# A float32 pipeline of attention and two weighted layers: six places for the row tiles of w_out, and a new order of seeds and sums at the borders and in the later experts

## The chip, the core and the metric

The kernel runs on one core of a Trainium2 chip. The metric is the device time of one execution in microseconds. The engines are named as in the profile: PE is the matrix engine (PEld its weight loads), DVE the vector engine, ACT the scalar engine, SP the queue from which all transfers are issued.

## The reference

Attention within chunks of 64 positions gives a matrix x of 2304 tokens by 512. A gated layer follows, and then four experts, weighted by probabilities:

```python
x = attention(q, k, v)                       # softmax(q k^T / 8) v, in chunks of 64
x = (x @ w_a * (x @ w_b)) @ w_out            # 512 -> 1536 -> 512
p = probs / (probs.sum(-1) + 1e-9)
for e in range(4):
    out += p[:, e] * (relu(x @ w1[e]) @ w2[e])   # 512 -> 1024 -> 512
```

All of it is float32. The 2304 tokens are worked in three thirds of 768.

## The kernel before

**Precision.** Each float32 operand is split into a rounded part (HI, written by ACT with a copy) and the rest (LO, written by DVE with a subtraction, line 1610). A product is three matmuls, lines 664 to 666: HI x HI, HI x LO, LO x HI. So an operand costs one ACT and one DVE pass before PE may read it, and the semaphores `..._hi` and `..._lo` count these passes.

**Fewer products.** Most stages multiply 2x2 blocks with seven products instead of eight, in an order that shares sums between the products. The names S1 to S4, XS1 to XS4 and T1 to T4 are sums of blocks. Partial results that two outputs share are copied from one PSUM bank to another, by ACT; these copies are the **seeds** (`seed_b`, `seed_c`, and in the later experts the copy that counts `x_seed`). PE waits for a seed before it adds a product on top of it.

**Stages of a third (T = 0, 1, 2).** Attention; six pairs `make_pair` of column blocks of w_a and w_b (14 groups of six matmuls each, 14.6 us); the layer w_out (`first_x2` in the first third, `later_x2` in the others); eight windows w = 0 to 7 of experts, two for each expert.

**The layer w_out in the first third, `first_x2`.** It uses twelve row tiles of w_out, i = 0 to 11, 24 matmuls for each, and adds all into eight PSUM banks. For each tile, ACT rounds the tile (`round_wo`) and the matching activations (`round_g`), and DVE writes the rests (`low_wo`, `low_g`; counters `wo_lo` and `gs_lo`). PE's tile i waits for `wo_lo` and `gs_lo` of i + 1. The later thirds use the seven-product form of w_out. The first third makes the pieces for it and stores them in DRAM: for each group u of four tiles, DVE forms four sums (`sum_wo`, lines 1816 to 1821) in the tiles `wo_three` and `wo_lone`, ACT and DVE split them, and SP stores them (`store_wo_sums`, four transfers of 512 KB). `sum_wo(u)` for u > 0 waits for `wot_kept`, the landing of the stores of group u - 1, because the place is one. The tiles themselves have three places, `wo[:, i % 3]`; `round_wo(i)` waits for PE's step i - 3 (`x2_step`) and for the store of tile i - 3 (`wo_kept`). The raw tiles come through four slots of `raw[:, 1]`, which the first expert's w2 (`load_w2(0)`) reuses.

**The border from T = 0 to T = 1.** Window 7 of the first third (`first_phase(7)`) also prepares operands of the next third: `round_sum` on ACT, `low_sum` and `sum_x` on DVE, for XA22, XS1, XA11, XS3, XS2, XA12, XS4.

**Pair 5 of the later thirds** also prepares the first operands of `later_x2`: `round_unit` on ACT; `low_unit` and `sum_g(T, XS3, u)` on DVE, for u = 0, 1, 2.

**The later experts, `later_phase(T, w)` and `make_out`.** The second product of a window has seven blocks on PE, in the order A22, A11, S1, S3, S2, A12, S4 (operands `hw`; results o4, o1, o5, o7, o6, o2, o3 in PSUM). Block 4 (S2) adds onto banks 2 and 3 and waits for `x_seed`, ACT's copy of banks 0 and 1 to banks 2 and 3. DVE takes results out of PSUM (counter `evac`, names a4, a7, a5, u, c11, a53). In windows 0 to 5 of T = 1, PE also makes attention scores between blocks 5 and 6, into banks 6 and 7, after ACT has cleared them (`cleared`, after a7 is out).

The order of work on each engine is the order in which it is written; each engine's queue is taken in that order, and a waiting instruction holds all behind it.

Of the kernel before, what the change touches and what calls it, by code (L numbers as in the profile page):

```python
# [12 lines left out]
P = 128  # L13
# [20 lines left out]
XS1, XS4, XA22, XA11, XA12, XS3, XS2 = range(7)  # L34
# [13 lines left out]
EVAC = ("a4", "a7", "a5", "u", "c11", "a53")  # L48
EVAC_LATE = ("a4", "a7", "a5", "a53", "u", "c11")
# [16 lines left out]
def build(nc, q, k, v, wab_in, wo_in, w1_in, w2_in, probs, out, out_t):  # L66
# [5 lines left out]
    with ctx:  # L72
# [49 lines left out]
        with ExitStack() as over:  # L122
            wo_three = sb(over, "wo_three", [P, 3, 2, 512], F32R)
            sb(over, "skip_wo_lone", [P, 2048])
            wo_lone = sb(over, "wo_lone", [P, 2, 512], F32R)
# [12 lines left out]
        with ExitStack() as over:  # L138
            wo = sb(over, "wo", [P, 3, 2, 512], F32R)
# [17 lines left out]
        with ExitStack() as over:  # L157
            sb(over, "skip_wo_b", [P, FA * 2 * N + 12 * N])
            wo_b = sb(over, "wo_b", [P, 3, 2, 512], F32R)
# [45 lines left out]
        def wos(i):  # L205

            return wo_b[:, i % WRING] if i % WRING < 3 else wo[:, i % WRING - 3]
# [69 lines left out]
        wo_kept = [sem(f"wo_kept{n}") for n in range(3)]  # L277
        wos_in = [sem(f"wos_in{n}") for n in range(WRING)]
# [55 lines left out]
        def evac_no(T, w, name):  # L334
            order = EVAC_LATE if T < NTH - 1 and w == PH - 1 else EVAC
            return 6 * no_w(T, w) + order.index(name) + 1
# [25 lines left out]
        def wo_stores(i):  # L362

            return sum(1 + (n % 4 >= 2) for n in range(i % 3, i + 1, 3))

        def wo_loads(T, i):

            return (T - 1) * len(range(i % WRING, UNIT3, WRING)) + i // WRING + 1
# [34 lines left out]
        def _(sp):  # L403
# [36 lines left out]
            def store_wo(i):  # L440
# [3 lines left out]
                for n, col in (((0, 0),) if i % 4 < 2 else ((3, 0), (6, 1))):  # L444
                    sp.dma_start(kept_wo[n, u, :, :, kt, :],
                                 wo[:, i % 3, :, col * 256:(col + 1) * 256].bitcast(F32)).then_inc(wo_kept[i % 3], 16)

            def store_wo_sums(u):
                sp.wait_ge(wot_lo, 2 * u + 2)
                for n, c in ((4, 0), (1, 1), (2, 2)):  # L450
                    sp.dma_start(kept_wo[n, u].rearrange("p z t n -> p z (t n)"),
                                 wo_three[:, c].bitcast(F32)).then_inc(wot_kept, 16)
                sp.dma_start(kept_wo[5, u].rearrange("p z t n -> p z (t n)"),
                             wo_lone[:, :].bitcast(F32)).then_inc(wot_kept, 16)

            def load_unit(T, i):
                sp.dma_start(wos(i).bitcast(F32),
                             kept_wo[i // 3, i % 3].rearrange("p z t n -> p z (t n)")).then_inc(wos_in[i % WRING], 16)
# [37 lines left out]
            def first_stage():  # L496
# [13 lines left out]
                for i in range(FA):  # L510
                    store_wo(i)
                    u = i // 4
                    if i == 3:
                        sp.wait_ge(wot_sum, 4)
                        for n in range(4, 8):
                            load_wo(n)
                        store_wo_sums(0)
                    if i == 6:
                        sp.wait_ge(wot_sum, 8)
                        for n in range(8, 11):  # L520
                            load_wo(n)
                    if i == 7:
                        load_wo(11)
                        store_wo_sums(1)
                        sp.wait_ge(p3_made, 2 * set_e(0, 0))
                        load_qk(TILES)
                        load_v(TILES)
                store_wo_sums(2)

            def later_stage(T):  # L530
# [6 lines left out]
                for j in range(PLAIN if T == 1 else 1, NPAIR):  # L537
                    for n in range(7):
                        if 7 * j + n >= RING:
                            load_block(T, j, n)  # L540
                        if (j, n) == (4, 4):
# [4 lines left out]
                            for p in range(3):  # L546
                                sp.wait_ge(wo_kept[p], 16 * wo_stores(FA - 3 + p))
# [15 lines left out]
            def first_windows():  # L563

                load_w2(0)
# [36 lines left out]
            def later_windows(T):  # L602
# [39 lines left out]
                if T == NTH - 1:  # L642
                    for name, n in (("u", G4), ("u", G5), ("c11", G11), ("a53", G53)):
                        sp.wait_ge(evac, evac_no(T, PH - 1, name))
                        sp.dma_start(out_t[T - 1, n, :, :], acc_t[:, n].rearrange("p s n -> p (s n)")).then_inc(stored, 16)

# [5 lines left out]
            sp.wait_ge(stored, 16 * (TILES + 4 * (NTH - 1)))  # L652
# [9 lines left out]
        def _(pe):  # L662
# [140 lines left out]
            def first_x2():  # L803
# [3 lines left out]
                def step(i, bank):  # L807
                    hf, col = int(bank in (2, 6)), int(bank >= 4)
                    for d in range(2):
                        at = col * 256 + d * P  # L810
                        last = product(ps[:, bank + d, 0:N], lambda part: wo[:, i % 3, part, at:at + P],
# [31 lines left out]
            def later_x2(T):  # L843
# [3 lines left out]
                def make(n, banks, first):  # L847
                    for u in range(3):
                        i = 3 * n + u
                        pe.wait_ge(wos_in[i % WRING], 16 * wo_loads(T, i))  # L850
                        pe.wait_ge(gs_lo, gs_count(T, i))
                        for kt in range(2):
                            for s in range(2):
                                at = kt * 256 + s * P
                                last = product(ps[:, banks[s], 0:N], lambda part: wos(i)[:, part, at:at + P],
# [238 lines left out]
        def _(act):  # L1094
# [107 lines left out]
            def run_pair(T, j):  # L1202
# [7 lines left out]
                next_ab(0)  # L1210
                for s in range(2):
# [26 lines left out]
                if j == NPAIR - 1:  # L1238
                    for i in range(3):
                        if T == 0:  # L1240
                            round_wo(i)
                            round_g(i)
                        else:
                            round_unit(T, i)
# [16 lines left out]
            def round_wo(i):  # L1261
                act.wait_ge(wo_in_s[i % 4], 16 * (i // 4 + 1))
                if i >= 3:
                    act.wait_ge(x2_step, i - 2)
                    act.wait_ge(wo_kept[i % 3], 16 * wo_stores(i - 3))
                copy(wo[:, i % 3, HI, :], raw_wo(i)).then_inc(wo_hi, 1)

            def round_g(i):
                f = WO_ORDER[i]
                act.wait_ge(g_set, 4 * pair_no(0, f // 2 + 1)) if f >= 2 * PLAIN else None  # L1270
# [1072 lines left out]
```

## Time and profile before

| | us |
|---|---|
| median of 3 runs | 1209.89 (1209.49 to 1214.25) |
| the profiled execution | 1209.57 |
| its span, first to last instruction | 1207.8 |
| PE busy | 1181.4 (98%) |
| DVE busy | 859.0 (71%) |
| ACT busy | 500.0 (41%) |
| DMA, of 16 engines | 71% |
| mean granted clock of PE | 0.993 |

The profiled execution's own time lies 1.8 us above its span. PE's busy time counts matmuls that overlap in its pipeline, so it shows idle time well and slow stretches badly. The 40 slices of the page (30.2 us each) show nines for PE except in the first, around 150 to 200 us, and in the last.

### The profile page before, as it was taken

Reading aid. Unit: us, or ns where it says so; the run is one execution under the profiler, and the core shown is the slowest. Engines: PE = TensorE matmul, PEld = TensorE weight load, DVE = VectorE, ACT = ScalarE, POOL = GpSimd, SP = SyncE. Lnnn points to the kernel's source line nnn. Section 1 sums busy time; section 2 is a strip of 40 time slices with the busy share of each in tenths; the row PEclk is TensorE's granted clock in tenths of the full one; section 3 lists DMA queues with packets and bytes.
Section 4 is the critical chain, followed back from the end, with each engine's and each line's share of the span. In section 5 each row is a group of like instructions: output and inputs, shape, how many; then the busy total and the mean of one; then the engine's idle time right before and its main releaser. Section 6 shows DMA issues by size and latency. Waiting matters only on the chain. (4 is left out here: it accounts for less than half of the span.)

```text
span 1207.8 us, 18849 instructions
## 1 busy us (share of the span) xinstructions
PE 1181.4 (98%) x7648; PEld 1135.7 (94%) x7648; DVE 859.0 (71%) x1147; ACT 500.0 (41%) x868; POOL 0.7 (0%) x6
## 2 busy tenths in 40 slices
PE   8999979999999999999999999999999999999997
PEld 8999978898988889999999999999999999999997
DVE  5776669888778893257877777797336786666687
ACT  5555355544444543225434434444224433333332
POOL 0000000000000000000000000000000000000000
PEclk9999998999999999999999999999999999999999
DMA  7296595987777699839777776647893867676761
GB/s 264 88 359 235 188 320 222 356 319 302 300 301 274 283 391 351 303 123 366 274 276 275 259 267 260 236 184 264 255 364 142 330 262 266 252 266 251 260 243 53
DMA packets 75323, 319.56 MB, mean 265 GB/s; under 512 B 7324, under 2 KB 18148, under 8 KB 58852
## 3 DMA queue, kind: packets, MB, share of 16 engines
q1 hardware_dynamic: 75236, 318.35, 71.1%
q8 instruction: 61, 1.00, 0.3%
q14 instruction: 26, 0.21, 0.1%
HBM read 221.81 MB, written 96.51 MB: 264 GB/s over the span
## 5 line engine op out<-in xcount | busy, mean ns | idle before, releaser
L664 PE MATMUL ps<-x,wab 128*128 128x384 f32 x504 | 169.5, 336 | 3.2 <-DVE c L1719 2.7
L666 PE MATMUL ps<-x,wab 128*128 128x384 f32 x504 | 168.5, 334 | 0.0
L665 PE MATMUL ps<-x,wab 128*128 128x384 f32 x504 | 168.5, 334 | 0.0
L1096 ACT ACTIVATE hw<-xraw 128x768 fp32r<-128x768 f32 x112 | 93.2, 846 | 179.8 <-DVE xraw L2081 80.7
L1096 ACT ACTIVATE ps<-ps 128x384 f32<-128x384 f32 (+1 forms) x184 | 91.4, 501 | 161.9 <-PE ps L666 161.8
L664 PE MATMUL ps<-hw,w2s 128*128 128x384 f32 x448 | 153.1, 342 | 1.4 <-DVE hw L1610 0.5
L664 PE MATMUL ps<-x,w1s 128*128 128x384 f32 x448 | 150.9, 337 | 0.0
L665 PE MATMUL ps<-hw,w2s 128*128 128x384 f32 x448 | 150.0, 335 | 0.0
L666 PE MATMUL ps<-hw,w2s 128*128 128x384 f32 x448 | 149.9, 335 | 0.0
L666 PE MATMUL ps<-x,w1s 128*128 128x384 f32 x448 | 149.8, 334 | 0.0
L665 PE MATMUL ps<-x,w1s 128*128 128x384 f32 x448 | 149.7, 334 | 0.0
L1610 DVE TENSOR_TENSOR hw<-xraw,hw 128x768 fp32r<-128x768 f32 x112 | 105.6, 954 | 2.3
L664 PEld LDWEIGHTS ps<-x,wab 128*128 128x128 f32 x504 | 94.6, 188 | 4.5 <-DVE c L1719 3.3
L665 PEld LDWEIGHTS ps<-x,wab 128*128 128x128 f32 x504 | 94.6, 188 | 0.0
L666 PEld LDWEIGHTS ps<-x,wab 128*128 128x128 f32 x504 | 94.6, 188 | 0.0
L664 PEld LDWEIGHTS ps<-hw,w2s 128*128 128x128 f32 x448 | 84.0, 188 | 10.1 <-issue 9.7
L664 PE MATMUL ps<-x,w 128*128 128x384 f32 x224 | 77.1, 344 | 8.9 <-DVE x L1610 6.8
L664 PEld LDWEIGHTS ps<-x,w1s 128*128 128x128 f32 x448 | 84.1, 188 | 0.4
L665 PEld LDWEIGHTS ps<-hw,w2s 128*128 128x128 f32 x448 | 84.2, 188 | 0.0
L665 PEld LDWEIGHTS ps<-x,w1s 128*128 128x128 f32 x448 | 84.1, 188 | 0.0
L666 PEld LDWEIGHTS ps<-hw,w2s 128*128 128x128 f32 x448 | 84.1, 188 | 0.0
L666 PEld LDWEIGHTS ps<-x,w1s 128*128 128x128 f32 x448 | 84.1, 188 | 0.0
(195 smaller groups left out, 2272.0 us busy)
## 6 DMA issues: line engine op xcount, KB each, us to landing
wab<-kept_ab SPq DMA_DIRECT2D x70, 512.0 KB, 4.9
w1s<-kept_w SPq DMA_DIRECT2D x32, 1024.0 KB, 6.6
w2s<-kept_w SPq DMA_DIRECT2D x16, 2048.0 KB, 7.4
w1s<-kept_w SPq DMA_DIRECT2D x16, 1536.0 KB, 6.1
w2s<-kept_w SPq DMA_DIRECT2D x16, 1536.0 KB, 6.1
kept_ab<-wab SPq DMA_DIRECT2D x42, 512.0 KB, 5.2
raw<-in_w SPq DMA_DIRECT2D x16, 1024.0 KB, 10.5
kept_w<-w SPq DMA_DIRECT2D x16, 1024.0 KB, 12.8
```

Source lines behind the costliest of these rows:

```text
L664: pe.matmul(dst, stat(HI), mov(HI), start=first, stop=False, skip_group_check=True)
L665: pe.matmul(dst, stat(HI), mov(LO), start=False, stop=False, skip_group_check=True)
L666: return pe.matmul(dst, stat(LO), mov(HI), start=False, stop=last, skip_group_check=True)
L1096: return act.activation(dst, src, ACT.Copy)
L1610: return dve.tensor_tensor(dst, src, f32(hi), ALU.subtract)
```

## The change

In `first_x2` the row tiles get six places, `wo_b` (i % 6 below 3) and `wo_a`; `round_wo(i)` waits for PE's step i - 6 and the store of tile i - 6. The activations `gs` keep three places. A tile now lies in its place as [column half, HI or LO, 256], so that a stored half is one piece of 2 KB per partition and not two of 1 KB. In the three queues, `sum_wo`, `round_wo_sums`, `low_wo_sums` and the loads of the next tiles stand ahead of the work for tiles that PE needs later, tile 3 is rounded already in pair 5, and `load_w2(0)` stands ahead of the stores of tile 11 and of the last sums.

At the border to T = 1, ACT does `seed_b` ahead of the operands of the next third, and DVE does XA12 and XS4 after `low_h` of C21. In pair 5 of the later thirds ACT rounds the units ahead of the seeds, and DVE makes two of the three XS3 sums in pair 4 and the third ahead of the units. In the later experts ACT makes the seed before it rounds A12, the sum for S4 is formed with the opposite operand as target (in the place of H11, not H12), DVE makes S4's operand ahead of the evacuations a5 and a7, and a7 is taken out before a5 in windows with scores only. In the last window the last evacuation and its store go in two halves.

```diff
-EVAC = ("a4", "a7", "a5", "u", "c11", "a53")
-EVAC_LATE = ("a4", "a7", "a5", "a53", "u", "c11")
+EVAC = ("a4", "a5", "a7", "u", "c11", "a53")
+EVAC_SCORE = ("a4", "a7", "a5", "u", "c11", "a53")
+EVAC_LATE = ("a4", "a5", "a7", "a53", "u", "c11")
...
             def round_wo(i):
                 act.wait_ge(wo_in_s[i % 4], 16 * (i // 4 + 1))
-                if i >= 3:
-                    act.wait_ge(x2_step, i - 2)
-                    act.wait_ge(wo_kept[i % 3], 16 * wo_stores(i - 3))
-                copy(wo[:, i % 3, HI, :], raw_wo(i)).then_inc(wo_hi, 1)
+                if i >= WRING:
+                    act.wait_ge(x2_step, i - WRING + 1)
+                    act.wait_ge(wo_moved[i % WRING], 16 * wo_stores(i - WRING))
+                copy(wos(i)[:, :, HI, :], raw_wo(i).rearrange("p (c n) -> p c n", c=2)).then_inc(wo_hi, 1)
...
+                sp.wait_ge(wot_sum, 12)
+                sp.wait_ge(wo_lo, FA)
+                load_w2(0)
+                store_wo(11)
                 store_wo_sums(2)
...
                 hi(S2, H11)
-                act.wait_ge(gated, 4 * V + 4)
-                hi(A12, H12)
                 act.wait_ge(o1_made, 2 * V + 2)
                 act.wait_ge(evac, evac_no(T, w, "a4"))
                 copy(block_of(2), block_of(0)).then_inc(x_seed, 1)
+                act.wait_ge(gated, 4 * V + 4)
+                hi(A12, H12)
+                act.wait_ge(hs_sum, 4 * V + 4)
+                hi(S4, H11)
```

**DVE in `first_x2`, the end of it.** Before, from tile 10 on: the rows `wo` and `gs` are a tile and its activations, the four rows that write `wo_three` and `wo_lone` from `raw` are `sum_wo(2)`.

```order
L1610 TENSOR_TENSOR wo<-raw,wo 128x512 [waits wo_hi]
L1610 TENSOR_TENSOR gs<-g,gs 128x2x384 [waits gs_hi]
L1610 TENSOR_TENSOR wo<-raw,wo 128x512 [waits wo_hi]
L1610 TENSOR_TENSOR gs<-g,gs 128x2x384 [waits gs_hi]
L1816 TENSOR_TENSOR wo_three<-raw 128x512 [waits wo_in3,wo_in2,wot_kept,wo_in1,wo_in0]
L1817 TENSOR_TENSOR wo_three<-raw 128x512
L1819 TENSOR_TENSOR wo_three<-raw,wo_three 128x512 [waits wot_sum]
L1821 TENSOR_TENSOR wo_lone<-raw,wo_three 128x512 [waits wot_sum]
L1610 TENSOR_TENSOR wo<-raw,wo 128x512 [waits wo_hi]
L1610 TENSOR_TENSOR gs<-g,gs 128x2x384 [waits gs_hi]
L1610 TENSOR_TENSOR wo_three<-wo_three 128x3x512 [waits wot_hi]
L1610 TENSOR_TENSOR wo_lone<-wo_lone 128x512 [waits wot_hi]
```

After, from tile 10 on (its `low_g` stands in the row with x3, with those of tiles 9 and 11):

```order
L1640 TENSOR_TENSOR wo_a<-raw,wo_a 128x2x256 [waits wo_hi]
L1850 TENSOR_TENSOR wo_three<-raw 128x2x256 [waits wo_in3,wo_in2,wot_kept,wo_in1,wo_in0]
L1851 TENSOR_TENSOR wo_three<-raw 128x2x256
L1853 TENSOR_TENSOR wo_three<-raw,wo_three 128x2x256 [waits wot_sum]
L1855 TENSOR_TENSOR wo_lone<-raw,wo_three 128x2x256 [waits wot_sum]
L1640 TENSOR_TENSOR wo_three<-wo_three 128x6x256 [waits wot_hi]
L1640 TENSOR_TENSOR wo_lone<-wo_lone 128x2x256 [waits wot_hi]
L1640 TENSOR_TENSOR wo_a<-raw,wo_a 128x2x256 [waits wo_hi]
L1640 TENSOR_TENSOR gs<-g,gs 128x2x384 [waits gs_hi] x3
```

Before, the activations of tiles 9 and 10 stand ahead of `sum_wo(2)`; now those of tiles 9, 10 and 11 stand behind `sum_wo(2)`, which waits for `wot_kept`, and behind its splitting.

**ACT in window 7 of the first third.** `ps<-ps` waiting for `p1_made` is `seed_b`, `x<-xf_later` the operands of the next third, `w<-raw` the two halves of w2. Before:

```order
L1096 ACTIVATE three<-three_f 128x3x512 [waits wt_sum]
L1096 ACTIVATE lone<-lone_f 128x512
L1096 ACTIVATE x<-xf_later 128x768 [waits attended,xf_set]
L1096 ACTIVATE x<-xf_later 128x768 x2
L1096 ACTIVATE ps<-ps 128x384 [waits p1_made,added] x2
L1096 ACTIVATE w<-raw 128x1024 [waits w2_kept,out_made,raw_in1]
L1096 ACTIVATE t_sb<-ps 128x384 [waits p7_made,c2_set] x2
L1096 ACTIVATE w<-raw 128x1024
L1096 ACTIVATE ps<-ps 128x384 [waits p6_made,added] x2
```

After:

```order
L1100 ACTIVATE three<-three_f 128x3x512 [waits wt_sum]
L1100 ACTIVATE ps<-ps 128x384 [waits p1_made,added] x2
L1100 ACTIVATE lone<-lone_f 128x512
L1100 ACTIVATE x<-xf_later 128x768 [waits attended,xf_set]
L1100 ACTIVATE x<-xf_later 128x768
L1100 ACTIVATE w<-raw 128x1024 [waits w2_kept,out_made,raw_in1]
L1100 ACTIVATE t_sb<-ps 128x384 [waits p7_made,c2_set] x2
L1100 ACTIVATE w<-raw 128x1024
L1100 ACTIVATE x<-xf_later 128x768
L1100 ACTIVATE ps<-ps 128x384 [waits p6_made,added] x2
```

`seed_b` has passed `lone` and three operands; `seed_c` (the last row) still stands behind all of them.

**ACT in a window of the later experts** (T = 2). `hw<-xraw` waiting for `gated` is A12, `ps<-ps` waiting for `o1_made` is the seed. Before:

```order
L1096 ACTIVATE hw<-xraw 128x768 [waits gated] x2
L1096 ACTIVATE hw<-xraw 128x768 [waits hs_sum] x3
L1096 ACTIVATE hw<-xraw 128x768 [waits gated]
L1096 ACTIVATE ps<-ps 128x2x384 [waits evac,o1_made]
L1096 ACTIVATE hw<-xraw 128x768 [waits hs_sum]
```

After:

```order
L1100 ACTIVATE hw<-xraw 128x768 [waits gated] x2
L1100 ACTIVATE hw<-xraw 128x768 [waits hs_sum] x3
L1100 ACTIVATE ps<-ps 128x2x384 [waits evac,o1_made]
L1100 ACTIVATE hw<-xraw 128x768 [waits gated]
L1100 ACTIVATE hw<-xraw 128x768 [waits hs_sum]
```

The seed now stands ahead of A12.

## Rows read from the trace of the kernel before

**Rows 1.** The page, its first line

```profile
span 1207.8 us, 18849 instructions
```

**Rows 2.** Waits of PE: engine, line, waited for; us in total, times, longest

```profile
PE ps L664 <- DVE x L1610: 6.8, 2, 5.8
PE ps L664 <- DVE c L1719: 2.7, 2, 1.3
PE ps L664 <- ACT ps L1096: 2.6, 2, 2.1
...
PE ps L664 <- DVE gs L1610: 1.8, 2, 1.2
PE ps L664 <- DVE h L1946: 1.4, 1, 1.4
```

**Rows 3.** Timeline of PE, first third: start, length, what [idle before <-releaser]

```profile
150.03 0.41 PE L664 MATMUL ps<-gs,wo 128*128 128x384 f32 x1 [0.58 <-DVE gs L1610]
...
181.71 0.69 PE L664 MATMUL ps<-x,w 128*128 128x384 f32 x1 [5.77 <-DVE x L1610]
...
182.83 0.52 PE L664 MATMUL ps<-x,w 128*128 128x384 f32 x1
183.15 0.52 PE L665 MATMUL ps<-x,w 128*128 128x384 f32 x1
...
190.69 0.33 PE L664 MATMUL ps<-x,w 128*128 128x384 f32 x1
...
191.73 0.33 PE L664 MATMUL ps<-x,w 128*128 128x384 f32 x1
```

**Rows 4.** Timelines of DVE, SP and ACT in the first w_out layer

```profile
121.70 0.55 DVE L1733 TENSOR_TENSOR g<-ps,a_sb 128x384 f32<-128x384 f32 x1
...
145.79 0.69 DVE L1816 TENSOR_TENSOR wo_three<-raw 128x512 f32<-128x512 f32 x1 [3.08 <-DMA kept_wo<-wo_lone]
...
166.30 1.76 DVE L1610 TENSOR_TENSOR wo_three<-wo_three 128x1536 fp32r<-128x1536 f32 x1 [0.42 <-ACT wo_three L1096]
...
164.80 1.47 ACT L1096 ACTIVATE wo_three<-wo_three 128x1536 fp32r<-128x1536 f32 x1
...
178.47 1.06 ACT L1096 ACTIVATE w<-raw 128x1024 fp32r<-128x1024 f32 x1 [6.14 <-DMA raw<-in_w]
...
137.27 1.63 SPq L451 DMA_DIRECT2D kept_wo<-wo_three  x3
...
171.62 1.20 SPq L464 DMA_DIRECT2D raw<-in_w  x1
```

**Rows 5.** PE by stretches: length, busy (matmuls), granted clock, DMA share, GB/s

```profile
180.00:181.00 1.00, 0.00 (x0) 0.81 0.96 229
...
187.00:188.00 1.00, 1.00 (x6) 0.77 1.12 479
...
420.00:422.00 2.00, 2.00 (x8) 0.50 0.99 410
```

**Rows 6.** Timelines of ACT and DVE in window 7 of the first third

```profile
415.35 2.29 ACT L1096 ACTIVATE x<-xf_later 128x768 fp32r<-128x768 f32 x3
417.55 0.84 ACT L1096 ACTIVATE ps<-ps 128x384 f32<-128x384 f32 x2
...
424.83 0.95 DVE L1610 TENSOR_TENSOR x<-xf_later,x 128x768 fp32r<-128x768 f32 x1
...
430.42 1.23 DVE L1946 SCALAR_TENSOR_TENSOR h<-c,h 128x384 fp32r<-128x384 f32 x2
```

**Rows 7.** Timeline of DVE, pair 5 of the second third

```profile
528.73 0.96 DVE L1610 TENSOR_TENSOR gs<-g,gs 128x768 fp32r<-128x768 f32 x1 [6.87 <-ACT gs L1096]
```

**Rows 8.** Timelines of ACT and PE, a window of the later experts

```profile
1045.47 0.79 ACT L1096 ACTIVATE ps<-ps 128x768 f32<-128x768 f32 x1
...
1046.37 0.41 PE L664 MATMUL ps<-hw,w2s 128*128 128x384 f32 x1
```

**Rows 9.** Timeline of DVE, its last row

```profile
1201.91 1.81 DVE L2092 TENSOR_TENSOR acc_t<-ps,acc_t 128x768 f32<-128x768 f32 x2
```

More of the change, by code:

```diff
@@ L31 @@
 B11, T3, B21, B22, T1, T2, T4 = range(7)
-XS1, XS4, XA22, XA11, XA12, XS3, XS2 = range(7)
+XS1, XS4, XA22, XA11, XA12, XS2, XS3 = range(7)
 XA21 = XS4
@@ L334, in evac_no @@
         def evac_no(T, w, name):
-            order = EVAC_LATE if T < NTH - 1 and w == PH - 1 else EVAC
+            order = EVAC if T == NTH - 1 else EVAC_SCORE if w < TILES else EVAC_LATE if w == PH - 1 else EVAC
             return 6 * no_w(T, w) + order.index(name) + 1
@@ L853, in make @@
                             for s in range(2):
-                                at = kt * 256 + s * P
-                                last = product(ps[:, banks[s], 0:N], lambda part: wos(i)[:, part, at:at + P],
+                                last = product(ps[:, banks[s], 0:N], lambda part: wos(i)[:, kt, part, s * P:(s + 1) * P],
                                                lambda part: gs[:, i % 3, part, kt, :], first and u == 0 and kt == 0,
@@ L1210, in run_pair @@
                 next_ab(0)
+                if T and j == NPAIR - 1:
+                    for i in range(3):
+                        round_unit(T, i)
                 for s in range(2):
@@ L1237, in run_pair @@
                     seed_c(Q, s)
-                if j == NPAIR - 1:
+                if T == 0 and j == NPAIR - 1:
                     for i in range(3):
[L1240 to L1244, printed above, removed]
+                        round_wo(i)
+                        round_g(i)
+                    round_wo(3)
                 next_ab(4)
@@ L1344, in split_w2 @@
                     act.wait_ge(raw_in[1], 16 * (3 + w + 1))
+                    if w == 0:
+                        for i in range(FA - WRING, FA):
+                            act.wait_ge(wo_moved[i % WRING], 16 * wo_stores(i))
                     if w:
@@ L1580, in _ @@
                 else:
-                    for i in range(3, FA):
-                        round_wo(i)
+                    round_wo_sums(0)
+                    round_g(3)
+                    round_wo(4)
+                    round_wo(5)
+                    round_g(4)
+                    round_wo(6)
+                    round_g(5)
+                    round_wo(7)
+                    round_wo_sums(1)
+                    round_g(6)
+                    round_g(7)
+                    round_wo(8)
+                    round_wo(9)
+                    round_g(8)
+                    round_wo(10)
+                    round_wo_sums(2)
+                    round_wo(11)
+                    for i in range(9, FA):
                         round_g(i)
-                        if i in (4, 7, 11):
-                            round_wo_sums((i - 3) // 3 if i < 11 else 2)
                     for n in range(3):
```

227 lines of the change are left out of this document (131 added, 96 removed).

## The prediction

> **What bounds the kernel now.** I read the page first: PE is busy in 98% of a span of 1207.8 us [rows 1], so the kernel can only gain what PE idles or loses to a low clock. The list of PE's waits [rows 2] comes next, and then PE's timeline around each of them. At full clock, six matmuls take 1.04 us, 0.1733 each (190.69 to 191.73) [rows 3], so any larger distance between starts is loss, also where no idle is printed. The losses are: in the first w_out layer and right behind it, 0.6 at 150.03, 1.2 us one row tile before its end, 1.1 and 5.8 at the start of the first expert [rows 2, 3]; the 5.8 comes with a clock at half from about 180.8 to 187.4 [rows 5], where matmuls stand 0.32 apart [rows 3]. At the border to the second third 2.1 us for a seed, followed by half clock around 420 [rows 2, 5], and 1.4 for `h`. In pair 5 of both later thirds 1.3 each. In each of the 16 windows of later experts, at block 4, a distance of 0.40 and then 0.25 in place of 0.17: 0.30 us; the late start stands 0.11 behind the end of ACT's seed at 1046.26 [rows 8].
>
> **The first w_out layer.** A tile is 24 matmuls, 4.16 us. I follow the three queues of the new order with the durations of before.
>
> DVE's last product of pair 5 stood at 121.70 [rows 4]. Tile 3 is now rounded ahead of it, one ACT pass (0.5) and one DVE pass (0.6) more, so it ends at 123.4. These also hold two products that PE's tile 0 needs for free banks: 0.2 us of new wait. `sum_wo(0)` follows at once: four passes 2.6, ACT's rounding 1.5, DVE's rests 2.4, so SP issues the sums of group 0 at 129.9, not at 137.27 [rows 4]. Their landing took 8.5 (145.79, where DVE had waited for it, less 137.27) [rows 4]; 129.9 + 8.5 = 138.4. Now `sum_wo(1)` waits for that with the activations of tile 6 behind it. 138.4 + 6.5 = 144.9 is the next issue; tile 6's activations end 0.9 later, at 145.8, where PE wants them at 145.3: 0.6 of new wait. 144.9 + 8.5 = 153.4 lets `sum_wo(2)` go. Behind it stand 2.6 of sums, 1.5 on ACT [rows 4], 1.7 and 0.6 of rests, 0.6 for tile 11 and only then 0.95 for the activations of tile 9: 161.4.
>
> PE came to tile 9 at 150.03 + 2 x 4.16 = 158.35 before [rows 3]. It loses the wait of 0.75 and gets 0.2 and 0.6: 158.4. So it waits **3.0 us at tile 9**, longer than any wait that the change removes inside this layer. Three tiles of 12.5 follow: the layer ends at 173.9, against 172.2 before (158.35 + 12.5 + 1.4 for the wait one tile from its end). Taken alone, the six places lose 1.7 us.
>
> What pays is the start of the expert. The load of w2 was issued at 171.62 and ACT could take it at 178.47 [rows 4], 6.85 later. It is now issued when tile 11's rest is done, at 160.5, and lands by 167.4. SP's queue behind it (tile 11's store, the sums, w1) is not wanted before 175: 3.7 MB from 161.4 at the 0.4 MB per us of [rows 5] (410 and 479 GB/s) is 9 us, 171 with the landing 172 to 173. ACT and DVE have the operand of S3 at 174.6. PE ends A11 at 173.9 + 2.1 = 176.0 and starts S3 without a wait; both the 1.1 and the 5.8 are gone, S2 may wait 0.1 for its seed: 176.1. Before, S3 started at 181.71 with 17 matmuls at 0.32 before the clock was back: 17 x 0.147 = 2.5, worth a start at 184.2. **Gain 8.1.** Against it stands the clock: an idle of 2.07 us was followed by half clock at the border [rows 2, 5], one of 1.4 (there and in the pairs) was not, and here are 3.0 in one piece. One such fall lasted 3.4 us at the border, 10.7 matmuls x 0.147 = 1.6. I take it as likely and leave **6.5**.
>
> The pieces of 2 KB in place of 1 KB: the DMA share is 0.96 to 1.12 in all stretches of [rows 5], whatever is in flight. I take nothing, and allow 1 us each way through the landings.
>
> By the Trainium skill, page "DMA: Bandwidth & Descriptors", section "Anatomy of one DMA", a transfer costs about 2.0 us plus its bytes over 436 GB/s, 6.8 us for the four sums. The trace has 8.5, since other transfers share the engines; by the page's figure both landings would come 1.7 earlier, the wait at tile 9 would shrink from 3.0 to nothing and the time would be that of the first rival.
>
> **The border.** ACT rounded three operands from 415.35 and seeded at 417.55 [rows 6]; PE had wanted the seed at 415.84. Now the seed runs at 414.8. But the second seed (`seed_c`) stands behind lone 0.5, two operands 1.5, w2 0.95, two saves 0.75, w2 0.95 and one operand 0.75, 5.4 in all from 415.6: done at 421.5 where PE comes at 420.0. That is a new wait of 1.5. Then DVE decides: it came to `low_h` after the operand at 424.83 and one more sum, and ended C21 at 431.65 [rows 6]; those two (1.86) now stand behind C21, so PE starts its second half at 429.9, not 431.8. **Gain 1.9**, whatever the seed brings; at least 0 (if DVE gets no further ahead), at most 3.8 (if DVE didn't bind).
>
> **Pair 5, twice.** DVE waited for ACT until 528.73 [rows 7], then did six passes of 0.87 ahead of the products that PE waits for. ACT's rounding now stands ahead of the seeds, at 520.6 to 522.9, and seeds PE still 1.9 in time; DVE's passes end by 525.5 in what was idle. 1.34 and 0.17 of slow restart: **3.0** for both.
>
> **Later experts.** ACT's seed started at 1045.47 behind A12 [rows 8]; a pass earlier it starts with the end of a4, 1044.85, and ends 0.4 before PE wants it (1046.1). Next late: S2's rest, done 0.2 to 0.3 ahead; A12's rest, which now comes one sum later, 0.4 ahead; in score windows the clearing after a7, two passes later, within 0.1; c11 for the next window 0.1 ahead. So 0.30 x 15 = **4.5**, since the last window ends on DVE. Bounds: nothing, if one of these slips; 4.8 with all.
>
> **The tail.** DVE runs nearly without idle to its last row [rows 9]. The last window has the same passes with two more dependent steps (0.3), halves cost 0.1 more, and the last half lands earlier: **-0.3**. The 0.5 wait of PE there buys nothing.
>
> Sum: 6.5 + 1.9 + 3.0 + 4.5 - 0.3 = 15.6. From the profiled execution's 1209.6 (span and 1.8 around; the median is 0.3 above) this gives **1194.0**.
>
> **Rivals.** (1) *The stores land early.* If the landings take 7 and not 8.5, both count: `sum_wo(2)` is released 3 us sooner, tile 9 hardly waits, no clock falls: 3.0 + 1.6 less, **1189.4**. For it: fewer, larger pieces; against it: the same bytes follow the sums in SP's queue as before. (2) *The experts give nothing*: in 16 windows margins of 0.1 to 0.4 decide, and if A12's rest or the clearing takes the seed's place as last, 4.5 are gone: **1198.5**. For it: DVE is the fuller engine there; against it: each margin came out above zero. (3) *Slower.* DVE now stands still at `sum_wo` with nothing that PE needs done ahead of it, so every us of landing counts twice. If the landings take 16 us instead of 8.5, tile 9 starts 15 us later, and with a further fall of the clock the 15.6 are gone: **1211**. It decides from some 16 us; the landing seen is 8.5, so it is remote. (4) The first layer brings half (another operand behind the w2 load is late at the expert's start), with a fall of the clock at the border's idles of 1.5 and 1.6: 1202.
>
> **How the numbers follow.** A measurement tells from no change what is more than 0.5%, 6 us: faster is below 1203.8. Chances: forecast 0.55, (1) 0.2, (2) 0.13, (4) 0.08, (3) 0.04. The range reaches from 1188, a little below (1), to 1199.5, above (2); outside are (3), (4) and little else. All but (3) and a part of (4) are faster: 0.93, same 0.04, slower 0.03.
>
> **What would show it.** In the profile after: one wait of about 3 us for `gs` some 161 us in, followed by half clock, the layer's end near 174, no wait at the first expert's S3; at the border waits of 1.5 for a seed and 1.6 for `h` in place of 2.1 and 1.4; no waits for `c` in pair 5; full pace at block 4 in the later windows. The forecast falls if DVE reaches `sum_wo(2)` without waiting for the landing, if w2 is still the last operand of the first expert, or if block 4 waits for `hw`.

## The result, and the profile after

The kernel after takes **1191.4 us** (median, 1191.03 to 1192.56) where the one before takes 1209.8: a ratio of 0.984, 95% interval 0.982 to 0.9865. Forecast was 1194.0 with 1188 to 1199.5 around it. The profiled execution took 1192.56 with a span of 1190.8, against 1209.6 and 1207.8 [rows 1]: 17.0 us less.

The waits of PE in the kernel after (engine, line, what it waited for; us in total, times, longest), to be read against [rows 2]:

```profile
PE ps L670 <- DVE gs L1640: 2.7, 1, 2.7
PE ps L688 <- DVE early L1674: 2.1, 1, 2.1
PE ps L670 <- ACT ps L1100: 1.8, 2, 1.3
PE ps L670 <- DVE h L1980: 1.6, 1, 1.6
```

The 6.8 us for `x` and the 2.7 us for `c` are gone; one wait of 2.7 for `gs` is new. The second row stands in the first 15 us, which the change doesn't touch.

The first w_out layer in the timelines of SP, DVE, ACT and PE, to be read against [rows 3, 4] (start, length, engine, line, what, [idle before <-releaser]):

```profile
128.64 1.58 SPq L453 DMA_DIRECT2D kept_wo<-wo_three  x3
142.90 2.18 SPq L453 DMA_DIRECT2D kept_wo<-wo_three  x3
158.68 0.33 SPq L463 DMA_DIRECT2D raw<-in_w  x1
160.01 2.10 SPq L453 DMA_DIRECT2D kept_wo<-wo_three  x3
...
136.33 0.69 DVE L1850 TENSOR_TENSOR wo_three<-raw 128x512 f32<-128x512 f32 x1 [2.51 <-DMA kept_wo<-wo_lone]
151.45 0.69 DVE L1850 TENSOR_TENSOR wo_three<-raw 128x512 f32<-128x512 f32 x1 [1.64 <-DMA kept_wo<-wo_lone]
158.50 2.69 DVE L1640 TENSOR_TENSOR gs<-g,gs 128x768 fp32r<-128x768 f32 x3
...
170.94 1.05 ACT L1100 ACTIVATE w<-raw 128x1024 fp32r<-128x1024 f32 x1
...
159.60 0.66 PE L670 MATMUL ps<-gs,wo_a 128*128 128x384 f32 x1 [2.70 <-DVE gs L1640]
```

The stores of the sums leave at 128.64 and 142.90; DVE goes on 7.7 and 8.55 us later, when they have landed. The activations of tiles 9 to 11 come behind all that, at 158.50, and PE has waited 2.7 us for them. w2 is asked for at 158.68, not 171.62, and ACT takes it at 170.94 with no wait.

PE by stretches (length, busy (matmuls), granted clock, DMA share, GB/s) behind that wait:

```profile
158.00:160.00 2.00, 0.40 (x1) 0.85 0.51 53
160.00:162.00 2.00, 2.00 (x8) 0.50 0.65 209
162.00:164.00 2.00, 2.00 (x11) 0.79 0.95 267
```

The clock stands at 1.2 GHz, half, for some three us.

The border and the end, from the timelines of PE, ACT and DVE, to be read against [rows 6] and [rows 9]:

```profile
413.10 0.44 PE L670 MATMUL ps<-x,w 128*128 128x384 f32 x1 [1.28 <-ACT ps L1100]
421.52 0.47 PE L670 MATMUL ps<-w,h 128*128 128x512 f32 x1 [1.55 <-DVE h L1980]
...
412.55 0.87 ACT L1100 ACTIVATE ps<-ps 128x384 f32<-128x384 f32 x2
...
420.14 1.23 DVE L1980 SCALAR_TENSOR_TENSOR h<-c,h 128x384 fp32r<-128x384 f32 x2
...
1034.88 0.95 DVE L2127 TENSOR_TENSOR acc_t<-ps,acc_t 128x768 f32<-128x768 f32 x1
...
1035.97 0.41 PE L670 MATMUL ps<-x,w1s 128*128 128x384 f32 x1
1036.22 0.33 PE L671 MATMUL ps<-x,w1s 128*128 128x384 f32 x1
...
1185.71 1.01 DVE L2236 TENSOR_TENSOR acc_t<-ps,acc_t 128x384 f32<-128x384 f32 x2
```

### Lengths of stretches

PE never rests long, so the start of its first product of each phase cuts an execution into stretches that can be compared between kernels. Each number below is the difference of two such starts in PE's timeline (start, the first: the time of the w_out layer's first product; tail: from the first product of the last window's second half to the end of the span). Most untouched stretches repeat within 0.1 us from kernel to kernel, so this tells far smaller things than the time of an execution does. The start, the w_out layer and the border window don't: the kernel after, run twice, has 54.36 and 53.23 us for the layer and 18.21 and 18.79 for the border window.

```
kernel            start   w_out  to 2nd half  border  pairs*   windows  windows  tail
                          layer  of expert 1  window  T=1      T=1      T=2
before            120.17  53.45  24.03        20.15   89.03    249.51   221.87   22.0
after             119.29  54.36  15.66        18.21   87.38    247.07   220.41   22.5
e1_w2_first       123.34  53.48  21.06        20.20   89.00    249.38   221.75   22.0
e2_old_order      123.04  51.58  24.44        18.29   87.39    247.09   220.44   22.5
e3_w2_late        124.04  54.26  15.69        18.48   87.38    247.10   220.44   22.5
e4_tile9          120.51  49.92  18.78        18.80   87.38    247.07   220.44   22.5
e5_seed_c         119.28  52.78  15.68        17.99   87.39    247.05   220.32   22.6
e6_seed_c_sums    119.53  54.16  15.67        15.62   88.33    247.06   220.39   22.5
e7_first_expert   119.20  49.96  16.54        18.23   87.39    247.08   220.42   22.5
e8_a7_last        123.96  54.26  15.67        18.65   87.39    247.06   219.65   22.5
e9_old_experts    120.55  55.83  15.66        18.39   87.39    249.36   221.71   22.1
e10 (two undone)  119.45  55.77  15.68        20.35   89.01    247.05   220.35   22.5
e11_after_again   119.75  53.23  15.67        18.79   87.38    247.12   220.42   22.5
e12_best          118.71  49.95  16.54        16.06   87.39    247.05   219.68   22.5
* from the second third's first product to its w_out layer, six pairs
```

The six pairs of the last third, not in the table, take 89.80 us before, 88.15 after and 89.80 in e10. The first column is work that no edit touched, but for tile 3's rounding at its end. It varies by 5 us, by idle time and the clock in the first 30 us (last section). So the times of executions scatter by some us, and I read each experiment by its stretches first and give its median beside them. All ratios are against the kernel before on the same chip.

### The profile page after: what moved, and what is told of

Read it like the earlier page. It is cut to its first block, busy times and chain, and to the rows that moved or that the text cites. A ratio compares the mean times of both kernels' runs of the same rounds, so it can differ in the third digit from the quotient of the medians.

```text
span 1190.8 us, 18862 instructions
## 1 busy us (share of the span) xinstructions
PE 1172.9 (98%) x7648; PEld 1131.8 (95%) x7648; DVE 860.6 (72%) x1148; ACT 502.0 (42%) x868; POOL 0.7 (0%) x6
## 4 chain that ended last, share of the span: by engine, by line
PE 88%; DVE 5%; DMA 3%; ACT 2%; issue 1%; SPq 1%; DVEq 0%; ACTq 0%
PE ps L670 29%; PE ps L672 28%; PE ps L671 28%; DMA kept_w<-w 1%; DMA kept_wo<-wo_lone 1%; PE ps L680 1%; PE ps L699 1%; PE ps L707 1%; PE ps L688 1%; DMA kept_w<-lone 1%; DVE wo_three L1640 0%; ACT wo_three L1100 0%; PE ps L743 0%; DVE x L1640 0%; SPq L453 0%
## 5 line engine op out<-in xcount | busy, mean ns | idle before, releaser
L670 PE MATMUL ps<-w,h 128*128 128x512 f32 x192 | 76.1, 397 | 1.6 <-DVE h L1980 1.6
```

Of the source, the lines that this page charges most:

```text
L670: pe.matmul(dst, stat(HI), mov(HI), start=first, stop=False, skip_group_check=True)
```

## Experiments

### The first layer: places, order, or w2's early load

**e1_w2_first**: the kernel before with

```diff
+                    if i == 10:
+                        sp.wait_ge(wot_sum, 12)
+                        sp.wait_ge(wo_lo, FA)
+                        load_w2(0)
                 store_wo_sums(2)
...
-                load_w2(0)
```

> The kernel before, with three places for row tiles and all its orders as they were, and one thing changed: the load of w2 is issued as soon as the rest of tile 11 is taken (164.9 in the trace of before), not behind the sums' stores (171.62). Theory (the early load pays, the six places do not): it lands 6.85 later, at 171.7; ACT rounds its half by 173.3 and S3's operand by 175, DVE has the rest of it at 176.4, so the wait of 5.8 at 181.71 shrinks to under 1 and the low clock behind it goes: 5.5 to 7.5 us faster than before, 1202 to 1204. Rival (six places and the new order of sums are needed): within 1.5 us of before, 1208 to 1210, the wait for x at the first expert still over 4 us.

Measured: 1204.2 us, ratio 0.996 (0.9945 to 0.997), 5.4 us under before, just short of my 5.5 to 7.5. Its profiled execution is the slowest of ten, 1209.59 us; its start takes 3.2 us more than before's, and the layer and the first half of the expert are 74.5 us against 77.5. The wait of 5.8 went, and two others came. PE, DVE and SP:

```profile
179.60 0.44 PE L667 MATMUL ps<-x,w 128*128 128x384 f32 x1 [0.44 <-DVE x L1613]
185.08 0.58 PE L667 MATMUL ps<-x,w 128*128 128x384 f32 x1 [3.10 <-ACT ps L1099]
...
182.11 0.96 DVE L1974 TENSOR_TENSOR xraw_b<-xraw 128x768 f32<-128x768 f32 x1 [1.70 <-DMA kept_wo<-wo_lone]
...
171.89 1.90 SPq L451 DMA_DIRECT2D kept_wo<-wo_three  x3
```

The seed of the third product waits for ACT, ACT for DVE, and DVE for the landing of the last sums' stores (issued at 171.89), whose place `xr(4)` takes. The old order sends these so late that they bind next; half clock followed. So the early load is worth something by itself (the second theory falls), but in the one execution that was traced it brings 2.9, half of what I gave it: I had not asked what is late behind w2. How much of the 5.4 by medians lies in these stretches and how much in the start can't be told from one trace.

**e2_old_order**: the kernel after with the old sequences of `first_x2` on ACT, DVE and SP, w2 loaded last; the six places stay.

> The kernel after, with its six places and shared semaphores, its border, pair 5 and experts, but in the first w_out layer the old order on ACT, DVE and SP: sums behind the tiles, loads behind the stores, w2 loaded behind the sums' stores. Theory (places alone buy little): only ACT's waits for kept_wo go; the sums' stores and w2 leave 1.5 to 2 us earlier than before, so this loses 5 to 7 us against after: 1196.5 to 1198.5. Rival (the places are the gain): within 2 us of after, 1191.5 to 1193.5.

Measured: 1200.9 us, ratio 0.993 (0.991 to 0.994). Layer and expert start take 76.0 us, 6.0 more than after (the rest of the difference lies in the start column). With the places and without the new order the layer is 1.9 shorter than before, since ACT no longer waits for the tiles' stores; the expert then waits 6.8 for w2, where before it waited 5.8. ACT in before (such a wait of 7.1 follows at 163.5), then ACT in e2:

```profile
146.42 0.63 ACT L1096 ACTIVATE wo<-raw 128x512 fp32r<-128x512 f32 x1 [7.99 <-DMA kept_wo<-wo]
...
180.51 1.06 ACT L1096 ACTIVATE w<-raw 128x1024 fp32r<-128x1024 f32 x1 [7.17 <-DMA raw<-in_w]
```

The theory held in the stretches, 6.0 where it had 5 to 7; the median is 9.5 above after's, with 3.7 more in the start of the traced execution. The new order was never tried with three places, so what it needs of them isn't shown.

**e3_w2_late**: the kernel after with

```diff
-                sp.wait_ge(wot_sum, 12)
-                sp.wait_ge(wo_lo, FA)
-                load_w2(0)
                 store_wo(11)
                 store_wo_sums(2)
+                sp.wait_ge(wot_sum, 12)
+                load_w2(0)
```

> The kernel after, with the one load of w2 put back behind tile 11's store and the four stores of the sums. Theory: the new order has those stores issued from 160.0 to 162.8, so w2 is issued near 163 and lands between 169.8 (6.85 later) and 172.5 (behind 2 MB of stores); ACT wants it at 170.9, so the loss against after is 0 to 1.5 us, taken as 0.8: 1192.2. Rival (its place in SP's queue ahead of the stores is what pays): 4 us or more lost, 1195.5 or above, with a wait for x in the first expert.

Measured: 1194.2 us, ratio 0.988 (0.987 to 0.990), but layer and expert start take 69.95 us, like after's 70.02; the profiled execution (1197.67) has 4.7 more than after's in the start. w2 was issued 43.4 us into the layer, 4.0 later than in after, and ACT still took it without a wait, 8.1 after the issue. So its jump over the stores bought nothing. **What brings w2 forward is the order of the sums**: before, the last sums' stores were issued 48.5 us into the layer, where their rests were done, and w2 behind them at 51.5; in e3 they leave at 40.0. In e2, with the old order, they leave at 46.7. SP in before, then SP in e3:

```profile
168.69 1.64 SPq L451 DMA_DIRECT2D kept_wo<-wo_three  x3
...
164.03 2.15 SPq L453 DMA_DIRECT2D kept_wo<-wo_three  x3
167.46 1.18 SPq L463 DMA_DIRECT2D raw<-in_w  x1
```

### Tile 9

**e4_tile9**: the kernel after, on DVE (on ACT alike)

```diff
                     low_wo(10)
+                    low_g(9)
                     sum_wo(2)
                     low_wo_sums(2)
                     low_wo(11)
-                    for i in range(9, FA):
+                    for i in range(10, FA):
                         low_g(i)
```

> The kernel after, with one step moved: the activations of row tile 9 are rounded and split ahead of the third group of sums on ACT and DVE. Theory: DVE stands still for the landing of the second group's stores at sum_wo(2) until 151.4 and reaches tile 9's rest behind it only at 158.5; moved ahead, it is there by 150, PE's wait of 2.7 at 159.6 and the half clock behind it (3 us in which columns cost double, 1.5 us lost) go; tile 10 becomes the next in line. DVE then ends the layer's sums 1 us later. Faster than after by 2 to 3.5 us, taken as 2.9: 1188.5. Rival (the layer is bound by DVE's sum of work there, so that the wait turns up at tile 10 or at x): within 0.5 us of after, 1191.

Measured: 1193.3 us (1188.96 to 1193.41), ratio 0.986 (0.984 to 0.988): no gain that a median shows. The stretches say why: the layer is 4.4 us shorter, with no wait and no half clock, and the first half of the expert 3.1 longer; 1.3 is left. PE, ACT and DVE:

```profile
173.35 0.44 PE L670 MATMUL ps<-x,w 128*128 128x384 f32 x1 [0.67 <-DVE x L1641]
177.96 0.44 PE L670 MATMUL ps<-x,w 128*128 128x384 f32 x1 [2.23 <-ACT ps L1100]
...
170.10 1.06 ACT L1100 ACTIVATE w<-raw 128x1024 fp32r<-128x1024 f32 x1 [2.28 <-DMA kept_wo<-wo_a]
...
174.99 0.96 DVE L2006 TENSOR_TENSOR xraw_b<-xraw 128x768 f32<-128x768 f32 x1 [0.82 <-DMA kept_wo<-wo_lone]
```

In after these landings were hidden behind the wait at tile 9. The theory did not have it. The rival had a wait turning up for `x`, and 0.67 of it did, but it came, like the 2.23, from landings and not from DVE's sum of work.

**e7_first_expert**: e4 with (shortened)

```diff
 # ACT                                   (DVE: the same, its w2 pass behind xr(3))
-                    split_w2(0, 0)
                     act.wait_ge(s_set, 1)
                     copy(x2[:, S3, HI], xr(2)).then_inc(x2_hi, 1)
+                    split_w2(0, 0)
 # DVE, ahead of xr(4)
-                dve.wait_ge(wot_kept, 64 * 3)
+                dve.wait_ge(wot_first, 16)
...
```

> The kernel after with tile 9's activations moved (as in the run e4_tile9), and three more edits at the start of the first expert: S3's operand ahead of w2's first half on ACT and DVE, w2's first half on DVE behind the sum xr(3), and xr(4) waiting for the landing of the first store of the last sums alone (the one whose place it takes), not for all four. Theory: in e4_tile9 the wait of tile 9 was replaced by two, 0.7 for S3's operand (ACT stood at w2 for the landing of row tiles' stores until 170.1) and 2.2 for the seed and S2 (DVE stood until 175.0 for the landing of the sums' stores); here the first goes and the second shrinks to 0.5 to 1.3: from the w_out layer's first product to the first expert's second half 66.5 to 67.5 us, where after has 70.0 and e4_tile9 68.7; total 2.5 to 3.5 us under after. Rival (all stores land together, so that naming the first one gains nothing): 68 us there.

Measured: 1189.8 us, ratio 0.983 (0.981 to 0.984); layer and expert start 66.5 us, 3.5 under after. No wait for S3's operand, one of 1.0 for the seed:

```profile
174.47 0.43 PE L674 MATMUL ps<-x,w 128*128 128x384 f32 x1 [0.99 <-ACT ps L1104]
```

DVE no longer waits for a landing there, nor does ACT ahead of w2. How much of the 2.2 us under e4 comes from the reorder and how much from naming the first store wasn't separated.

### The border

**e5_seed_c**: the kernel after, ACT's window 7 with

```diff
+                    seed_c(Q, s)
+                if w == PH - 1:
+                    split_w2(w, 1)
+                    round_sum(1, XA12)
```

in place of the order that has `seed_c` last.

> The kernel after, with ACT's second seed of the border window (T=0, w=7) ahead of w2's second half and the operand XA12, not behind them. Theory (my forecast of the border: the wait for the seed is harmless, DVE's late low_h decides the end): PE's wait of 1.3 at 413.1 goes, and the wait for h at 421.5 grows from 1.6 to 2.9: from the window's first product to its second half 18.2 us as before the edit, total unchanged, 1191.4. Rival (the two waits add up, as the list of waits suggests): 1.3 us faster, 16.9 us in that window.

Measured: 1192.3 us (1190.78 to 1192.85), ratio 0.984. The wait for the seed is gone, yet the window takes 17.99 us, and the eight traced executions in which it is as in after have 18.2 to 18.8. PE:

```profile
415.68 0.44 PE L670 MATMUL ps<-x,w 128*128 128x384 f32 x1 [1.29 <-DVE c L1750]
419.71 0.47 PE L670 MATMUL ps<-w,h 128*128 128x512 f32 x1 [1.55 <-DVE h L1981]
```

The 1.3 turned up two products later as a wait for DVE's `c`, and the wait for `h` stayed 1.55. Not where I had put it (I had said `h` would grow to 2.9), but the point stands: the seed was not what bound. The window is 0.2 shorter than the shortest of those eight and 0.5 shorter than their mean of 18.5, not 1.3.

**e6_seed_c_sums**: the same and

```diff
                         low_sum(1, XA22)
-                        sum_x(1, XS1)
                         low_sum(1, XA11)
                         split_w2(w, 0)
-                        sum_x(1, XS3)
-                        sum_x(1, XS2)
                         split_w2(w, 1)
...
                     low_sum(1, XA12)
-                    sum_x(1, XS4)
+                    for a in (XS1, XS3, XS2, XS4):
+                        sum_x(1, a)
```

> The kernel after with the edit of the run before, and on DVE the three sums XS1, XS3 and XS2 of the next third's operands (0.9 each) behind C21 in the border window. Theory: DVE reaches its first low_h 2.8 earlier, so both waits go: 18.2 becomes 15.3 to 15.7 us from the window's first product to its second half, 2.5 to 2.9 us faster than after, 1188.7. Rival (C12's rest or the sums for pair 0, now later on DVE, are wanted in time): the gain shows up again as a wait of over 1 us at the third or fourth row tile of the second half, or at pair 0 of the next third, and the total stays within 1 us of after.

Measured: 1192.5 us (1190.9 to 1196.16), ratio 0.986 (0.984 to 0.988). The window is 2.6 us shorter, as the theory has it, though a wait of 0.76 for `h` is left; the pairs behind it are 0.95 longer, as the second theory has it. That leaves 1.6 us of gain in the stretches, which the median doesn't show. PE waits at pair 0:

```profile
444.49 0.44 PE L670 MATMUL ps<-x,wab 128*128 128x384 f32 x1 [0.64 <-ACT ps L1100]
```

DVE has no idle of 1 us or more through the border, and its first pass behind the longest of them, 0.97, starts at 431.6, in after at 431.3, while PE comes 2.6 us earlier. So only the waits that hang on the order of its passes can be had there.

### The later experts and pair 5

**e9_old_experts**: the kernel after with the windows of T=1 and T=2 as before: `A12` ahead of `x_seed` on ACT; on DVE S4's sum behind `a7` and again in the place of H12, and `a7` ahead of `a5`.

> The kernel after, with the windows of the second and last third in the old order: S4's sum and rest behind a7 on DVE, the operand A12 ahead of x_seed on ACT, a7 ahead of a5. Theory (my term of 0.30 for each of 15 windows; in the trace of after the second third gained 0.30 to 0.33 a window, the last one a net 0.2): block 4 waits again for its seed in every window, 2.4 us more in the second third, 1.5 in the last: 3.9 slower than after, 1195.3; the segments outside these windows as in after. Rival (the windows' gain came from elsewhere, the clock or the landings): within 1 us of after, and windows of 31.4 us in the second third as in after, not 31.7.

Measured: 1197.1 us, ratio 0.989 (0.987 to 0.9905). ACT and PE in the third window of T=1:

```profile
657.71 0.79 ACT L1100 ACTIVATE ps<-ps 128x768 f32<-128x768 f32 x1
...
658.22 0.34 PE L672 MATMUL ps<-hw,w2s 128*128 128x384 f32 x1
658.60 0.41 PE L670 MATMUL ps<-hw,w2s 128*128 128x384 f32 x1
```

0.38 between two starts where 0.17 is full pace, and in after there is no such place. The windows of T=1 are 2.3 longer, those of T=2 1.3, and the tail is 0.4 *shorter*: 3.2 in sum, where I had 3.9. The gain is the order's, and so is a loss in the last window.

**e10_old_border_pair5**: both parts undone, in stretches of their own.

> The kernel after, with two parts undone that lie in separate stretches of the trace: the border window (operands ahead of the seeds, the lone operand's rounding in the window before, XA12's rest and XS4 ahead of low_h) and pair 5 of the two later thirds (roundings behind the seeds, XS3's sums between the rests). Theory: from the border window's first product to its second half 20.2 us where after has 18.2; pair 5 waits 1.3 for c again, 1.65 from each of the two last pairs: 5.2 us slower, 1196.6. Rival (each hides in the other: with the border undone, pair 0 or the next third takes up the slack): under 3.5 us.

Measured: 1198.4 us, ratio 0.990 (0.988 to 0.992). The border window has 20.35 and the two groups of pairs 1.63 and 1.65 more: 5.4. Each part pays its own.

**e8_a7_last**: the kernel after with the order a4, a5, u, c11, a7, a53 in seven windows of T=2 (shortened).

```diff
                 else:                    # windows w=0 to 6 of T=2
                     add_a5()
-                    add_a7()
...
+                if not (attention or final):
+                    add_a7()             # behind c11
```

> The kernel after, with DVE taking a7 behind c11 in the seven windows w=0 to 6 of the last third. Theory: there c11 ends 0.1 us too late for the next window's first product (ends 1035.83, and the distance of starts at 1035.97 is 0.27, not 0.17); one pass of 0.87 earlier it is in time, and each of the seven windows is 0.10 shorter: the last third from 947.9 to 1168.3 takes 219.7 us and not 220.4. Total 0.7 less. Rival (PE's loss there is not from c11 but from the change of instruction kind): nothing, 220.4.

Measured: 1194.6 us, ratio 0.986 (0.984 to 0.989); its start column has 123.96. The windows of T=2 take 219.65, 0.76 less. DVE's c11 and PE's next window:

```profile
1038.96 0.96 DVE L2128 TENSOR_TENSOR acc_t<-ps,acc_t 128x768 f32<-128x768 f32 x1
...
1040.84 0.33 PE L671 MATMUL ps<-x,w1s 128*128 128x384 f32 x1
1041.01 0.33 PE L672 MATMUL ps<-x,w1s 128*128 128x384 f32 x1
```

In after the same two starts stand 0.25 apart (1035.97, 1036.22), here 0.17.

### The yardstick, and a better kernel

**e11_after_again**: no edit.

> The kernel after, unchanged, as the yardstick of this chip. What both theories say: its stretches from the first w_out layer on agree with the first profile of it to 0.1 us, but for the wait at row tile 9 and the clock behind it (1.6 us more or less) and up to 0.5 in the border window; its start up to the w_out layer varies, 119.3 to 124 us by the clock and one idle of PE in the first 25 us, which by itself moves the total between 1190 and 1196.

Measured: 1193.8 us, ratio 0.987 (0.985 to 0.988), with the granted clock at 0.995 in three of four executions; in the first set of executions it was 0.997 to 0.999 and the median 1191.4. The stretches agree to 0.1 but for the three that the text names. So a median of four executions of this kernel is good to some 2 us, and nothing above that is smaller was read from medians.

**e12_best**: e7, e6 and e8 together, and on ACT in pair 0 of T=1 `save_t` and `seed_c` ahead of the roundings for pair 1.

> The parts that paid, together: the edits of e7_first_expert, e6_seed_c_sums and e8_a7_last, and, against the wait of 0.6 that e6 left at pair 0 of the second third, ACT's save and second seed of that pair ahead of its roundings for the next pair. Theory: the stretches add up, 3.5 (first w_out layer and expert), 2.6 (border), 0.75 (last third), and 0.9 that e6 gave back stays: 6.9 us under after in the stretches behind the start, 1184 to 1186 in time. Rival (with PE earlier at the border, DVE's full queue gives the gain back at pair 0): 1186.5 to 1188, with a wait of 0.6 or more near the first pair of the second third.

Measured: **1186.7 us** (1185.22 to 1187.46), ratio 0.980 (0.979 to 0.982), 7 us under the kernel after on the same chip. The stretches: layer and expert start -3.5, border -2.15, last third -0.7, and the pairs have 87.39: what e6 gave back is not lost here. One new wait of 0.5 for `h` stands in the second window of the first third, in the stretch that the table leaves out. That is 5.9 in sum, not 6.9. The median lies just above my 1184 to 1186 and within the rival's 1186.5 to 1188, but the wait that the rival had at pair 0 isn't there: the border window brings 0.4 less than in e6, and the new wait costs 0.5. The waits of PE that are left:

```profile
PE ps L693 <- DVE early L1687: 2.1, 1, 2.1
PE ps L675 <- ACT ps L1105: 1.5, 2, 1.0
PE ps L675 <- DVE h L1993: 1.4, 2, 0.9
```

## Why the prediction was right, step by step

It was right in size and, mostly, for its reasons: the terms' sum was 15.6, the traces give 17.0, of which 0.9 lies in the start and is luck: the start varies by 5 us. Without it the traces give 16.1. The median, 1191.4, lies 2.6 from the forecast and 2.0 from the first rival's 1189.4, so the number alone would not tell them apart; the landings and the wait at tile 9 do.

- **The chain of the sums in the first layer: right.** Forecast: stores at 129.9 and 144.9, landings of 8.5 each, tile 9's activations done at 161.4, a wait of 3.0. Measured: 128.64 and 142.90, 7.7 and 8.55, PE at tile 9 at 159.60 (forecast 161.4), a wait of 2.7. All of it is 1.3 to 2.0 early; 0.9 of that is the start. The 0.2 at tile 0 came out as 0.3 just ahead of the layer, at 117.1; the 0.6 at tile 6 didn't come. So the layer takes 54.4 us, the fall of the clock included, where the forecast comes to 55.3 (173.9 less 120.2, and 1.6 for the clock).
- **The clock: right in size, not certain.** I took 1.6 for half clock behind the wait. Less what the wait at tile 9 adds to the distance between two starts (2.87 in after), the layer takes 51.4 to 51.6 us where the clock fell (after, e3, e6, e8) and 50.05 where it did not (e5, e11), so a fall costs 1.3 to 1.6. With a longer spell at half clock (e9, e10) it is 52.8. The fall at the border of the kernel before, from which I took the 1.6, cost nothing there: the window has 20.15 us with it and 20.20 in e1, where a wait of 2.12 for the same seed was followed by full clock and by one more wait, of 1.1 for `c`.
- **The expert's start: right in size, half wrong in its cause.** 6.5 was forecast with the fall of the clock, 7.5 measured (77.48 less 70.02); most of the difference is the 0.6 at tile 6 that didn't come and the 0.3 less at tile 9. The step "it is now issued when tile 11's rest is done" named w2's early issue as what pays. e3 shows that its place ahead of the stores is worth nothing, e1 that w2 alone brings 2.9 in the profiled execution and 5.4 by medians, and that the landing of the last sums' stores is late right behind it. What pays is that the last sums' stores leave 8 us sooner (40.7 into the layer, before 48.5): w2 follows in time, and their places are free for `xr(4)`. "Taken alone, the six places lose 1.7 us" was put on the wrong part as well: by e2 the places alone shorten the layer by 1.9, and it is the new order that makes it 2.8 longer again.
- **The border: right.** 1.9 forecast, 1.94 measured (and 2.14 by e10; against the mean of the eight windows it is 1.7); the two waits of 1.5 and 1.6 came as 1.3 and 1.55, and e5 shows that the first is harmless.
- **Pair 5: right.** 3.0 forecast, 1.65 each, 3.3.
- **The later experts: a little over.** 4.5 forecast, 3.9 measured (2.44 in T=1, 1.46 in T=2; 3.6 by e9). The step that failed is the margin "c11 for the next window 0.1 ahead": it ended 0.14 before PE's next start, and that was too close: each window of T=2 lost 0.10 there. e8 gave it back.
- **The tail: right, a little under.** -0.3 forecast, -0.5 measured. e9 has the halves and the old order, and its tail is before's, 22.1 to 22.0: the halves give nothing and the order costs 0.4, where the forecast had 0.3 for its two dependent steps.
- **The rivals.** Early landings (1189.4): the first landing was 0.8 shorter, the second was not, and DVE waited for each. Experts that give nothing, and a slower kernel: no trace of either. The pieces of 2 KB, put at nothing, stand in e2 too, with the old order: its landings are 8.5 and 8.3, those of before 8.5 and 8.4.
- **The skill's figure.** By the Trainium skill, page "DMA: Bandwidth & Descriptors", section "Anatomy of one DMA — SWDGE (gpsimd) path", the four sums' stores would land in an estimated 6.8 us. The section gives its figure for transfers issued from the gpsimd engine; here SP issues them, which the prediction left out. The landings that DVE waited for took 7.7 and 8.55 in after, 8.5 [rows 4] and 8.4 in before, 7.3 to 9.7 in all runs, and none as little as 6.8. The measurement decides; 8.5 was a fair value to take.

## What to carry to other kernels

When a late load is cured, look up what else was issued late for the same reason: here w2 and the sums' stores stood behind one rest on DVE, and curing one alone gave a part. A wait on the engine that bounds the kernel hides the waits behind it (tile 9 hid two landings); take it away and read the next ones before counting the gain. And where buffers are released by the landing of a store, try to wait for the store that frees the piece you need, not for the whole group; in e7 this came together with a reorder, and its own share isn't known.

## What the runs showed of the hardware

**The start of the same instructions takes 118.7 to 124.0 us.** All kernels have the same work up to the w_out layer but for a few passes at its end. PE by stretches in e3_w2_late, where it took 124.04:

```profile
15.00:20.00 5.00, 4.45 (x111) 1.00 1.04 396
20.00:25.00 5.00, 2.50 (x21) 0.69 0.42 119
25.00:30.00 5.00, 5.00 (x48) 0.63 0.56 193
```

and in after, 119.29:

```profile
15.00:20.00 5.00, 4.45 (x119) 1.00 1.04 399
20.00:25.00 5.00, 4.90 (x83) 1.00 0.40 135
25.00:30.00 5.00, 5.00 (x58) 1.00 0.61 204
```

In e3 PE stood idle for 2.5 us near 21, waiting for nothing that the profile shows, and worked at half clock behind it. e1, e2 and e8 have such an idle too (2.3 to 2.5), and half clock behind it; all others have less than 1 us of it there. A third way is half clock between 13 and 17 us, as in before, e4 and e9; e2 has both. The instructions are the same in all, and why it comes one way or another stays open; no run was made for it.

**Behind an idle of 2 to 3 us half clock comes in some executions and not in others.** Of eight profiled executions with the wait at tile 9, six had half clock behind it (after 2.70, e3 2.52, e6 2.62, e8 2.47, e9 2.90, e10 2.78 us), two had none (e5 2.57, e11 3.01). Elsewhere 2.07 (before) and 2.29 us (e10) at the border were followed by half clock, 2.12 (e1, border) and 2.23 us (e4, first expert) were not, and no idle of 1.0 to 1.7 us behind the start was. The length of the idle doesn't tell them apart; what does stays open. PE in e11_after_again:

```profile
158.00:160.00 2.00, 0.00 (x0) 1.00 0.00 0
160.00:162.00 2.00, 1.60 (x9) 1.00 0.82 98
162.00:164.00 2.00, 2.00 (x14) 1.00 1.04 344
```
